# A three-stage kernel: row tiles and earlier weights in the last stage, tile 0 loaded ahead, another routing

## The reference

```python
noisy_logits = x @ w_gate + log1p(exp(x @ w_noise)) * noise
top2 = indices of the two largest; top2_w = their softmax
h = relu(x[mask] @ w1[e]); out[mask] += top2_w * (h @ w2[e])
```

```python
h = x @ w_in
solu = h * softmax(h)
ln = (solu - mean(solu)) / sqrt(var(solu) + 1e-6) * g_ln
return ln @ w_out
```

## Time and profile before

| what | value |
|---|---|
| median of 3 runs | 573.43 us |
| profiled execution | 573.77 us, span 572.0 us |
| PE busy | 530.2 us (93%) |
| DVE, ACT, POOL busy | 231.3, 133.3, 101.3 us |
| attention / routing / experts / last stage begin at | 19.4 / 94.8 / 119.3 / 433.5 us |
| DMA | 60.17 MB, mean 105 GB/s |

### The profile page before, as it was taken

The page is one execution under the profiler, slowest core; times in us unless marked ns, Lnnn a source line. Parts: engine busy times, 40 slices in busy tenths (PEclk is TensorE's granted clock), DMA queues, the critical chain, the costliest instruction groups (busy, mean ns, idle before and its releaser), DMA issues.

```text
span 572.0 us, 8709 instructions
## 1 busy us (share of the span) xinstructions
PE 530.2 (93%) x2663; PEld 356.4 (62%) x2664; DVE 231.3 (40%) x514; ACT 133.3 (23%) x280; POOL 101.3 (18%) x124
## 2 busy tenths in 40 slices
PE   2699995389999999999999999999998999999996
PEld 2699994266666666666666666666664565655654
DVE  6188795942131212213121221312115666566552
ACT  3445453001111111111111111111110233233232
POOL 2435440130011001001100100110025122122000
PEclk9799998589999999999999999999999999999998
DMA  5957853657777741101101100110045011111000
GB/s 168 290 168 237 254 177 119 217 146 242 235 245 231 228 138 43 32 25 50 37 25 39 45 31 25 50 37 25 11 116 191 28 46 57 34 46 57 11 24 23
DMA packets 33139, 60.17 MB, mean 105 GB/s; under 512 B 5584, under 2 KB 22320, under 8 KB 32992
## 3 DMA queue, kind: packets, MB, share of 16 engines
q1 hardware_dynamic: 24720, 42.77, 23.7%
q0 software_dynamic: 3136, 10.03, 6.3%
q10 hardware_dynamic: 5264, 7.12, 3.5%
HBM read 49.96 MB, written 9.95 MB: 105 GB/s over the span
## 4 chain that ended last, share of the span: by engine, by line
PE 79%; DVE 8%; DMA 6%; issue 3%; ACT 2%; SPq 1%; POOL 1%; POOLq 0%; DVEq 0%
PE ps_y L1179 22%; PE ps_lr L1158 10%; PE ps_a L1158 9%; PE ps_y L1230 9%; PE ps_a L1222 5%; PE ps_b L1168 5%; PE ps_lr L1222 5%; PE ps_lr L1148 3%; PE ps_a L1148 2%; DMA mb_sb<-m_dram 2%; PE ps_y L1097 2%; PE ps_b L1239 2%; PE ps_t L1135 2%; ACT decay L568 1%; DMA xg<-x_dram,token_idx 1%
## 5 line engine op out<-in xcount | busy, mean ns | idle before, releaser
L883 DVE COPY hT<-ps_b 128x512 f32<-128x512 f32 x86 | 55.4, 686 | 209.1 <-PE ps_b L1168 182.5
L1179 PE MATMUL ps_y<-w_sb,hT 128*128 x496 | 138.7, 433 | 0.5 <-issue 0.5
L1179 PEld LDWEIGHTS ps_y<-w_sb,hT 128*128 128x128 f32 x496 | 93.1, 190 | 42.8 <-issue 8.4
L490 POOL DMA_INDIRECT xg<-x_dram,token_idx x31 | 29.6, 955 | 244.7 <-PE ps_t L1135 239.7
L1158 PE MATMUL ps_a<-w_sb,xT 128*128 x128 | 57.7, 593 | 0.0
L1230 PE MATMUL ps_y<-wout_sb,hT 128*128 128x320 f32 x192 | 55.6, 444 | 1.9 <-DVE hT L883 1.9
L1158 PE MATMUL ps_lr<-w_sb,xT 128*128 x120 | 55.5, 605 | 0.0
L1230 PEld LDWEIGHTS ps_y<-wout_sb,hT 128*128 128x128 f32 x192 | 36.6, 195 | 16.9 <-DVE hT L883 2.4
L603 ACT COPY y_sb<-ps_y 128x320 f32<-128x320 f32 x31 | 13.2, 426 | 122.7 <-PE ps_y L1179 122.7
L1158 PEld LDWEIGHTS ps_lr<-w_sb,xT 128*128 128x128 f32 x120 | 21.6, 189 | 26.5 <-issue 26.5
L1158 PEld LDWEIGHTS ps_a<-w_sb,xT 128*128 128x128 f32 x128 | 23.1, 190 | 23.3 <-issue 23.3
(11 more groups left out here) (175 smaller groups left out, 542.2 us busy)
## 6 DMA issues: line engine op xcount, KB each, us to landing
w_sb<-w SPq DMA_DIRECT2D x8, 1280.0 KB, 6.4
w_sb<-w SPq DMA_DIRECT2D x16, 512.0 KB, 4.9
mb_sb<-m_dram SPq DMA_DIRECT2D x12, 512.0 KB
y_dram<-y_sb ACTq DMA_DIRECT2D x31, 160.0 KB, 1.8
kvo_sb<-kvo SPq DMA_DIRECT2D x12, 324.0 KB
qk_sb<-qk SPq DMA_DIRECT2D x24, 160.0 KB
w_sb<-w SPq DMA_DIRECT2D x16, 128.0 KB, 5.5
gate_o<-og ACTq DMA_DIRECT2D x1, 1920.0 KB, 7.6
```

The source lines that it names most:

```text
L490: pool.indirect_dma_start(out=xg[:, b % 2], out_offset=None, in_=x_dram, in_offset=bass.IndirectOffsetOnAxis(ap=token_idx[:, b:b + 1], axis=0)
L883: dve.tensor_copy(hT[:, n * 4:n * 4 + 4], ps_b[:, n].rearrange("p (k s) -> p k s", s=P)).then_inc(ready, 1)
L1179: last = pe.matmul(ps_y[:, 0:DM], hT[:, k], w.rearrange("p o n -> p (o n)"), start=(k == 0), stop=(k == FT - 1))
```

## The change

- Start: f and i gates are loaded by SP and ACT with their own semaphores; q, k, v of tile 0 are loaded before the scans; `mb` counts on a semaphore `mb_in` for which only POOL's mask waits; in tile 0 PE multiplies the identity twelve times ahead of the value product; POOL's loop over tiles is written out; the wait for the sigmoid stands ahead of the first use.
- Routing: ACT takes the absolute value from PSUM itself; the scan over tiles (of each token row's own choices, `upto`) is made ahead of the PE products, which add both into one PSUM array `before`; copy, subtraction and addition behind them go; `pick` is made in four operations of six matrices each.
- Last stage: its contraction is 128 + 128 + 64 as in the experts, with `tail_products` and an x2 of 384 columns (a second operation in `combine`); `xT` has two buffers; w_in and w_out get places of their own and are loaded behind the last expert's weights; POOL scales w_out before block 23's gather; tile 0's hidden layer is done in halves with turn_tile(1) between them; `out_layer` waits for the halves of hT singly; at the end the maxima and the softmax of tile 11 come ahead of copy_vT(10), and ACT's order changes with them.

```diff
@@ sync @@
-            sp.dma_start(f_row[:], gates[0]).then_inc(gates_in, 16)
-            sp.dma_start(i_row[:], gates[1]).then_inc(gates_in, 16)
+            sp.dma_start(f_row[:], gates[0]).then_inc(f_in, 16)
...
+            sp.wait_ge(zeroed, 1)
+            load(0, 0)
             sp.wait_ge(gate_rows, 4)
...
             load_mb(0, 0)
-            sp.wait_ge(zeroed, 2)
-            load(0, 0)
...
-            sp.wait_ge(b_hidden, 2 * NBLK + R)
-            for k, (k0, kn) in enumerate(KT):
-                sp.dma_start(win_sb[0:kn, k], w_in[k0:k0 + kn]).then_inc(win_in, 16)
+            sp.wait_ge(y_zeroed, 16 * UNREAD)
+            for k in range(KF):
+                sp.dma_start(win_sb[:, 2 * k:2 * k + 2], ...).then_inc(win_in, 16)
+            for n in range(2):
+                sp.dma_start(win_sb[ODD_TAIL * n:ODD_TAIL * (n + 1), 2 * KF], ...).then_inc(win_in, 16)
             sp.dma_start(wout_sb[:], ...).then_inc(wout_in, 16)
@@ gpsimd @@
-                    pool.wait_ge(tile_in[u], 64 * (it + 1))
+                pool.wait_ge(tile_in[u], 48 * (t // U + 1))
...
+                pool.wait_ge(mb_in[u], 16 * (t // U + 1))
                 pool.affine_select(out=mb_sb[:, u], ...).then_inc(masked, 1)
...
             for b in range(NBLK):
+                if b == NBLK - 8:
+                    pool.wait_ge(wout_in, 16)
+                    pool.wait_ge(small_in, 32)
+                    pool.tensor_tensor(wout_sb[:], wout_sb[:], g_sb[:]..., ALU.mult).then_inc(wout_scaled, 1)
@@ scalar @@
-            act.wait_ge(gates_in, 32)
+            act.dma_start(i_row[:], gates[1]).then_inc(i_in, 16)
             act.dma_start(gate_o[:], og).then_inc(og_in, 16)
...
+            act.wait_ge(logits_done, done(NT - 1))
+            act.activation(r1[:], lgp[:, :, E:2 * E], ACT.Abs).then_inc(route_act, 1)
+            act.wait_ge(route_act, 1)
+            act.activation(r1[:], r1[:], ACT.Exp, scale=-1.0).then_inc(route_act, 1)
...
             softmax(NT - 2, 0)
-            scale_out(NT - 3, 1, NT // 2 - 2)
             square(NT - 2)
             softmax(NT - 1, 1)
+            scale_out(NT - 3, 1, NT // 2 - 2)
+            square(NT - 1)
             scale_out(NT - 2, 0, NT // 2 - 1)
-            square(NT - 1)
             scale_out(NT - 1, 1, NT // 2 - 1)
@@ vector @@
-            dve.tensor_tensor(both[:], one1[:], one2[:], ALU.add).then_inc(route_sums, 1)
+            step(dve.tensor_tensor(both[:, :, 1:NT + 1].rearrange("p e t -> p t e"), one1[:], one2[:], ALU.add))
+            dve.tensor_tensor_scan(upto[:]..., seg[:]..., both[:]..., 0.0, ALU.mult, ALU.add).then_inc(route_sums, 1)
...
-            step(dve.tensor_copy(tot[:]..., ps_r[:, 128:128 + NT * E]...))
-            step(dve.tensor_tensor_scan(incl[:]..., seg[:]..., tot[:]..., 0.0, ALU.mult, ALU.add))
...
-            step(dve.tensor_tensor(upto[:], incl[:], tot[:], ALU.subtract))
-            step(dve.tensor_tensor(pos[:], upto[:]..., ps_r[:, 0:NT * E]..., ALU.add))
...
-            for n in range(2 * NT):
-                dve.tensor_scalar(pick[:, n], iota_ph[:], slot_p[:]...[:, n:n + 1],
-                                  None, ALU.is_equal).then_inc(pick_ready, 1)
+            for n in range(0, 2 * NT, GROUP):
+                dve.tensor_tensor(pick[:, n:n + GROUP], iota_ph[:].unsqueeze(1).broadcast_to([P, GROUP, P]),
+                                  slot_ph[:, n:n + GROUP].unsqueeze(2).broadcast_to([P, GROUP, P]),
+                                  ALU.is_equal).then_inc(pick_ready, 1)
...
-            dve.wait_ge(wout_in, 16)
-            dve.tensor_tensor(wout_sb[:], wout_sb[:], g_sb[:]..., ALU.mult).then_inc(wout_scaled, 1)
...
-            for t in (NT - 2, NT - 1):
-                solu(t, t % 2)
-                copy_vT(t)
-                variance(t)
+            solu(NT - 2, 0)
+            maxima(NT - 1, 1)
+            variance_at(NT - 2, ends3 + 6)
+            shift_by(NT - 1, ends3 + 5)
+            copy_vT(NT - 2)
+            product(NT - 1, 1)
+            centre(NT - 1, ends3 + 8)
+            copy_vT(NT - 1)
+            variance_at(NT - 1, ends3 + 9)
@@ tensor @@
+                if t == 0:
+                    keep_warm(12)
                 pe.wait_ge(prob_ready, done(t))
...
-            pe.matmul(ps_r[:, 0:NT * E], tri[:], chosen, start=True, stop=True).then_inc(route_sums, 1)
-            pe.matmul(ps_r[:, 128:128 + NT * E], ones[:], chosen, start=True, stop=True
+            pe.matmul(before, ones[:], upto[:], start=True, stop=False)
+            pe.matmul(before[:, :, 0:NT], tri[:], both[:, :, 1:NT + 1], start=False, stop=True
                       ).then_inc(route_sums, 1)
...
+            def in_tails(t, u):
                 pe.wait_ge(s_xT, done(t))
                 pe.wait_ge(s_mean, done(t - R))
-                for n in range(2):
-                    for k, (k0, kn) in enumerate(KT):
-                        last = pe.matmul(ps_hidden[u][:, n], xT[0:kn, 0, k], win_sb[0:kn, k, ...],
-                                         start=(k == 0), stop=(k == 2))
-                    last.then_inc(s_hidden, 1)
+                tail_products(ps_hidden[u], u, win_sb[:, 2 * KF])
+
+            def in_half(u, n):
+                for k in range(KF):
+                    last = pe.matmul(ps_hidden[u][:, n], xT[:, u, k], win_sb[:, 2 * k + n],
+                                     start=False, stop=(k == KF - 1))
+                last.then_inc(s_hidden, 1)
...
             def out_layer(t):
-                pe.wait_ge(s_vT, 2 * t + 2 + R)
                 pe.wait_ge(s_osb, done(t - 1))
                 for k in range(FT):
+                    if k % 4 == 0:
+                        pe.wait_ge(s_vT, 2 * t + k // 4 + 1 + R)
...
             turn_tile(0)
-            pe.wait_ge(win_in, 48)
-            in_layer(0, 0)
+            pe.wait_ge(win_in, 64)
+            in_tails(0, 0)
+            in_half(0, 0)
             turn_tile(1)
+            in_half(0, 1)
             in_layer(1, 1)
```

More of the change, by code:

```diff
@@ L50 @@
 LGN = 96
+GROUP = 6
 NEG = -1.0e30
@@ L166, in build @@
         slots_of = place("slots_of", [P, 2, NT, E])
-        both = place("both", [P, NT, E])
+        both = place("both", [P, E, NT + 1])
         em8 = place("em8", [P, E])
@@ L221, in build @@
         zeroed = sem("zeroed")
[L222 removed]
+        f_in = sem("f_in")
+        i_in = sem("i_in")
         og_in = sem("og_in")
@@ L237, in build @@
         tile_in = [sem(f"tile_in{u}") for u in range(U)]
+        mb_in = [sem(f"mb_in{u}") for u in range(U)]
         x_out = [sem(f"x_out{u}") for u in range(U)]
@@ L943, in _, with maxima @@
             base3 = steps[0] + LEAD
-            def solu(t, u):
+            def maxima(t, u):
                 for n in range(2):
@@ L981, in variance, with solu @@
                                          ).then_inc(s_var, 1)
+            def solu(t, u):
+                maxima(t, u)
+                shift_by(t, base3 + 5 * t + 2)
+                product(t, u)
+                centre(t, base3 + 5 * t + 3)
+            def variance(t):
+                variance_at(t, base3 + 5 * t + 4)
             def copy_vT(t):
@@ L1126, in turn_rows @@
             def turn_rows(src, turned):
-                for k, (k0, kn) in enumerate(KT):
-                    last = pe.transpose(ps_t[0:KR, k * P:(k + 1) * P], src[:, k0:k0 + KR], ident[:])
+                for k in range(KF + 1):
+                    last = pe.transpose(ps_t[:, k * P:(k + 1) * P], src[:, k * P:(k + 1) * P], ident[:])
                 last.then_inc(turned, 1)
@@ L1133, in turn_block, with tail_products @@
                 pe.wait_ge(b_xT, done(b - 1))
-                for k in range(KF + 1):
-                    last = pe.transpose(ps_t[:, k * P:(k + 1) * P], xg[:, u, k * P:(k + 1) * P], ident[:])
-                last.then_inc(b_turned, 1)
+                turn_rows(xg[:, u], b_turned)
             def expert_of(b):
                 return pe.value_load(block_expert[0:1, ds(b, 1)], min_val=0, max_val=E - 1)
+            def tail_products(hidden, u, weights):
+                for q in range(2):
+                    for n in range(2):
+                        rows = slice(ODD_TAIL * n, ODD_TAIL * (n + 1))
+                        last = pe.matmul(hidden[:, n, q * QUART:(q + 1) * QUART], xT[rows, u, KF],
+                                         weights[rows, q * QUART:(q + 1) * QUART], start=(q == 0), stop=False)
+                return last
             def tails(b, u):
@@ L1144, in tails @@
                 pe.wait_ge(b_xT, done(b))
-                for q in range(2):
-                    for n in range(2):
-                        rows = slice(ODD_TAIL * n, ODD_TAIL * (n + 1))
-                        last = pe.matmul(ps_hidden[u][:, n, q * QUART:(q + 1) * QUART], xT[rows, u, KF],
-                                         tail_sb[rows, u, q * QUART:(q + 1) * QUART], start=(q == 0), stop=False)
-                last.then_inc(b_tails, 1)
```

(1 more changed line is left out.)

190 lines of the change are left out of this document (96 added, 94 removed).

## The result

The changed kernel took 556.59 us (median of 4 runs, 553.82 to 557.41) against 573.35 us before (4 runs, 573.13 to 574.19): ratio 0.970, 95% interval 0.966 to 0.973. Timed again beside the experiments it took 556.28 us (6 runs), ratio 0.968, interval 0.964 to 0.972. The forecast was 556.1 us. Each stage runs from where the one above it ends; all times are read from the two timelines.

The account below looks back on a forecast made before the run. PE bounds the kernel, with 79% of the chain of waits. Start -5.3, routing -0.45, turn -3.0, cycles -4.2 and end -4.4 sum to -17.35: 573.77 becomes 556.4, against the median 556.1 us; range 552.5 to 560.5.

Parts of the forecast that it names:

- The cycle: Last stage, nine cycles: hidden layer 4.69 us for 5.16 through paired 64-row products, -0.47 each, -4.2 us in all.
- The turn: From experts to last stage: faster y gather, hidden layer in halves, scaling off DVE; -3.0 us, bounds -1.3 to -3.6.
- VectorE's scaling: Turn to the last stage: tile 0's maxima stood behind DVE's 2.8 us scaling of wout, which the change removes.
- GpSimd's scaling: Experts: POOL scales wout before gather 23 in 2.7 to 5.5 us, free below 10 us.
- The start: Start of the attention: earlier mask and warm value product at 22.4 us; -5.3 us, bounds -2.3 to -6.3.
- the stall of tile 8: Attention: tile 8's value product waited 0.27 us for DVE, its logits as long; this goes, -0.5 us.
- Rival (b): Start gives half: mb lands with its followers, or the twelve warming products run at the lower level; 559.1 us, chance 0.17.
- The routing: Routing: fewer small DVE steps -1.2 us, against +0.75 for picks in four groups; -0.45 us.
- PE then needs its 3.85 again: Routing: PE starts later behind grouped picks and takes 3.85 us for 24 products as before; part of +0.75 us.
- The end: Last tiles: earlier softmax, half-wise waits and a faster closing product; -4.4 us, the cycle's 0.47 included, bounds -2.7 to -4.6.
- PE's gaps getting shorter: The end: gaps shrink from about 1 to 0.5 us, so the closing product takes 4.57 us and not 6.26.
- The sum: Whole kernel: all parts together -17.35 us, 573.77 becomes 556.4, against the median 556.1 us; chance 0.53.

Follow-up runs that it names:

- single_tails: Changed kernel with the last stage's 64-row products not in pairs, one of 512 columns ahead of each half's 128-row products; 569.82 us, ratio to before 0.992.
- late_weights: Changed kernel with last-stage weights loaded only after the last block's hidden layer, w_out scaled by VectorE behind tile 0's xT copy; 559.09 us.
- before_again: The kernel before the change, unchanged, profiled and timed once more; 573.84 us.
- start_undone: Changed kernel with q, k, v of tile 0 loaded behind mb again and without the twelve warming products; 559.37 us.
- whole_waits: Changed kernel, but out_layer waits for both halves of the copied hidden rows before its first product; 557.72 us.
- picks_one_by_one: Changed kernel with 24 single tensor_scalar picks instead of four operations of six; 555.90 us.
- end_old: Changed kernel with the old order of the last two tiles on VectorE and ScalarE, and out_layer waiting for both halves; 557.47 us.

## Why the prediction was right, step by step

- **The cycle** (-4.2 forecast, -4.21): a set of four 64-row products costs 0.86 and a change of tiling 0.20. single_tails bears out both terms with one more set and two more changes per cycle. The Trainium skill (TensorEngine Tiling (Array Packing), "Key Properties") says that a change of tiling mode drains the engine. The 0.20 us agree, in the experts, in the last stage and in single_tails.
- **The turn** (-3.0, -3.25): the transposes start 1.04 us sooner against the last expert product (1.3 forecast), and from there to tile 0's hidden turn it is 2.21 less (1.8). late_weights bears out the first: with the late load the transposes start 2.0 us later. For the second the size was right and the reason wrong. The prediction has the maxima wait for VectorE's scaling, but in the kernel before VectorE had scaled and combined by 439.01 and sat idle for 1.46 us until PE's transposes of tile 1:

```profile
440.47 0.56 DVE L877 COPY xT<-ps_t 112x384 f32<-112x384 f32 x1 [1.46 <-PE ps_t L1128]
```

These stood behind the whole hidden layer of tile 0, and behind them the copy and the combining of tile 2, so that the maxima began 1.7 us after that layer's end (440.11, 441.82). In the changed kernel turn_tile(1) stands between the two halves, and the maxima begin 0.1 before the layer's end (432.39, 432.52). That gives 1.8 of the 2.2, the shorter layer the rest; what the scaling's move gives is not shown, beyond the estimate of 0.8 at late_weights. No run undoes the halves alone. GpSimd's scaling took 4.46 us, inside the bounds of 2.7 to 5.5, and hidden. In before_again the same stretch takes 21.5 us, 2.6 more than in the profile of before (1.7 of it the clock, 0.9 a later gather), so the gain is 3.3 or 5.9 by which profile is taken.
- **The start** (-5.3, -4.19): the way was right (mask, value product, warm scores in the forecast order). Three sizes were off: mb landed near 17.9 and not 17.2, as its issue was not unchanged (start_undone has it back at 12.52); tile 1's value product had a new wait of 0.79 (up to 1.32 in other profiles, none in some); and the stall of tile 8, which I let go for 0.5, stayed (0.22).
- **Rival (b)**, the warming products at the lower level, is no rival but happens in a share of the executions. In three of ten profiles of kernels with this start the clock rose only in the second warming, and the value product came at 24.50 to 25.89. In whole_waits, whose edit is 400 us later:

```profile
21.23 4.82 PE L1054 MATMUL ps_lr<-ident 128*128 128x128 f32 x24
25.89 1.95 PE L1126 MATMUL ps_y<-kvo_sb,prob 128*128 128x123 f32 x16
```

- **The routing** (-0.45, -1.42): the failed term is "PE then needs its 3.85 again". The row of 3.85 us for 24 products in the earlier trace rows was VectorE's pace of 0.16 us a pick; PE's own is 0.08. Sent in groups of six, PE fits between them. The picks cost -0.18 and not +0.75; the rest (-1.2) came as forecast: from the logits' end to slot_bh 12.59 us became 11.34. The Trainium skill (SBUF — State Buffer, "Who interferes with whom") says that a VectorE instruction with two inputs in SBUF contends with a GpSimd instruction that reads SBUF, and that the order of issue decides which of the two waits. The trace agrees twice: behind VectorE's first group of six GpSimd's product took 2.08 us, where it took 1.44 with single picks (picks_one_by_one), and the 8-element step took 1.02 us within a mask of 1.09, where 0.17 is its time alone.
- **The end** (-4.4, -4.27): the sum is right and one term is not the change's. 0.47 are the cycle, 2.1 are order and half-wise waits, about 1.7 are the closing product, 6.26 before and 4.55 after. I had laid that to PE's gaps getting shorter. end_old has the old gaps and 4.57; before_again is the old kernel and has 4.57. Without this luck of the profile of before, the end would have given -2.6. Whether the medians hold such a loss can't be read from them. The mean granted clock of single runs is 0.961 to 0.982 in the kernel before and 0.978 to 0.982 in the changed one: there is less time at the lower level after the change, but not every such loss is placed. What decides when one comes remains open.
- **The last 0.45 of the routing** and the experts' -0.13 were forecast as nothing; the first is the warming between gather and transposes at a higher clock for longer (4.80 for 5.24 us), which varies from profile to profile.
- **The sum** came within 0.5 us of the median, and that is in part luck: the start gave 1.1 us less than forecast and the routing with its last part 1.4 more.

## What to carry to other kernels

A group of instructions on an engine that is fed one by one shows its feeder's pace: before a duration is called an engine's own, look for the same operation when all its inputs are there. An operation that stands ahead of a late one is not for that its cause: ask what the engine waited for in between. A stretch at a lower clock in one profile is not a property of that place until a second profile has it too; don't count it as the gain of an edit near it. When a transfer is moved forward, ask what small round trip now has to share the DMA with it.

## What the runs showed that was not expected

- A clock loss of about 1.7 us stands in the closing product in one profile of the kernel before and not in the next, with the same work and the same gaps there. In tile 0's hidden layer it stands in the two profiles in which PE had waited 1.83 and 1.87 us for the y rows, and in none of the other twelve.
- With the same instructions until then, the clock had risen before the twelve warming products in seven of ten profiles, and rose only within them in three. The value product starts at 22.50 to 23.05 us in the seven, 1.5 to 3.4 us later in the three.
- A 64-row product alone costs as much (1.05 us to the next product's start) as two side by side (1.06), and one of 512 columns as two of 256.
- A step of VectorE on 8 elements a row took 1.02 us while GpSimd masked 1024 a row; in eight of the twelve tiles it takes 0.17.
